# First-batch attention of a fused attention and MoE kernel: second q/k buffers, pooling on TensorE, and another order of the turns

## What is computed

```python
q_d = q.reshape(B, H, Sd, 4, D).mean(axis=3)     # k_d, v_d likewise
out_up = np.repeat(sm_attn(q_d, k_d, v_d), 4, axis=2)
mask = np.abs(pos[:, None] - pos[None, :]) < 4
attn = softmax(where(mask, scale * q @ k.T, -1e9))
x = (out_up + attn @ v).transpose(0, 2, 1, 3).reshape(1152, 512)
h = x @ w_in;  g = where(h > 0, h, exp(min(h, 0)) - 1);  x = g @ w_out
out = sum_e p[:, e] * (relu(x @ w1[e]) @ w2[e])
```

## Time and profile before

| | us |
|---|---|
| runs | 667.95, 667.06, 668.51; median 667.95 |
| profiled execution | 667.47, of which 665.4 are the span |
| start of the first pooled scores of pairs 0, 1 | 9.01, 16.96 |
| start of mix for pairs 0, 1, 2, 3 | 23.27, 32.20, 40.98, 47.49 |
| first layer-1 product, turn_in(4) | 49.18, 54.04 |

### The profile page before, as it was taken

The page is one execution under the profiler, slowest core; times in us unless marked ns, Lnnn a source line. Parts: engine busy times, 40 slices in busy tenths (PEclk is TensorE's granted clock), DMA queues, the critical chain, the costliest instruction groups (busy, mean ns, idle before and its releaser), DMA issues.

```text
span 665.4 us, 12923 instructions
## 1 busy us (share of the span) xinstructions
PE 651.9 (98%) x4750; PEld 599.6 (90%) x4756; DVE 324.4 (49%) x714; ACT 277.7 (42%) x759; POOL 304.5 (46%) x266
## 2 busy tenths in 40 slices
PE   7989999999999999999999999999999999999998
PEld 4768999999999999999989998998899899899886
DVE  4785454545444433465525435544454454365342
ACT  3766565656565653745214214233142162142110
POOL 3584343535359733878716326326138056061110
PEclk9999999999999999999999999999999999999999
DMA  9945070705112132111101103003003011010012
GB/s 181 242 74 163 4 199 4 196 1 162 66 53 76 65 104 84 64 64 65 64 1 64 65 0 123 3 0 126 0 13 113 0 63 63 1 64 0 1 48 95
DMA packets 51489, 46.11 MB, mean 69 GB/s; under 512 B 31616, under 2 KB 33920, under 8 KB 51456
## 3 DMA queue, kind: packets, MB, share of 16 engines
q1 hardware_dynamic: 51456, 45.67, 23.2%
HBM read 43.30 MB, written 2.36 MB: 69 GB/s over the span
## 4 chain that ended last, share of the span: by engine, by line
PE 88%; ACT 5%; DVE 5%; issue 1%; POOL 0%; ACTq 0%; DVEq 0%
PE psum L437 19%; PE psum L439 18%; PE psum L438 18%; PE psum L516 9%; PE psum L518 9%; PE psum L514 9%; ACT attn L670 2%; ACT attn_p L670 1%; DVE neg_max L901 1%; PE psum L355 1%; PE psum L342 1%; PE psum L429 1%; PE psum L408 1%; PE psum L374 1%; DVE sums L911 1%
## 5 line engine op out<-in xcount | busy, mean ns | idle before, releaser
L1162 POOL TENSOR_TENSOR wb_lo<-wb_raw,wb_hi 128x512 fp32r<-128x512 f32 x64 | 82.2, 1298 | 202.4 <-ACT wb_hi L702 202.4
L1028 DVE SCALAR_TENSOR_TENSOR o_acc<-psum,gate_now,o_acc 128x512 f32<-128x512 f32 x72 | 54.1, 751 | 125.6 <-PE psum L439 125.3
L439 PE MATMUL psum<-wb_hi,h_lo 128*128 128x512 f32 x288 | 112.3, 390 | 0.0
L438 PE MATMUL psum<-wb_lo,h_hi 128*128 128x512 f32 x288 | 112.2, 390 | 0.0
L437 PE MATMUL psum<-wb_hi,h_hi 128*128 128x512 f32 x288 | 112.0, 389 | 0.0
L759 ACT ACTIVATE h_hi<-psum 128x320 fp32r<-128x320 f32 (+1 forms) x128 | 52.4, 411 | 87.8 <-DVE psum L1000 40.4
L1162 POOL TENSOR_TENSOR wa_lo<-wa_raw,wa_hi 128x512 fp32r<-128x512 f32 x60 | 76.0, 1294 | 22.6 <-ACT wa_hi L746 14.1
L765 ACT COPY sums<-psum 128x256 f32<-128x256 f32 (+1 forms) x32 | 12.8, 400 | 156.4 <-PE psum L518 156.4
L437 PE MATMUL psum<-h_hi,wb_hi 128*128 128x288 f32 x256 | 76.8, 300 | 0.0
L439 PE MATMUL psum<-h_hi,wb_lo 128*128 128x288 f32 x256 | 75.4, 295 | 0.0
L438 PE MATMUL psum<-h_lo,wb_hi 128*128 128x288 f32 x256 | 75.4, 294 | 0.0
(11 more groups left out here) (146 smaller groups left out, 1539.4 us busy)
## 6 DMA issues: line engine op xcount, KB each, us to landing
wa_raw<-in_moe_w_in SPq DMA_DIRECT2D x8, 1024.0 KB, 5.7
wb_raw<-in_moe_w_out SPq DMA_DIRECT2D x8, 1024.0 KB, 5.1
wa_raw<-in_moe_w SPq DMA_DIRECT2D x8, 1024.0 KB, 4.9
wb_raw<-in_moe_w SPq DMA_DIRECT2D x8, 1024.0 KB, 5.0
out<-o_acc SPq DMA_DIRECT2D x9, 256.0 KB, 2.0
q_in<-in_q SPq DMA_DIRECT2D x10, 144.0 KB, 3.6
k_in<-in_k SPq DMA_DIRECT2D x10, 144.0 KB, 4.2
v_in<-in_v SPq DMA_DIRECT2D x5, 288.0 KB
```

The source lines that it names most:

```text
L438: nc.tensor.matmul(bank_cols, w_hi(n), x_lo_(n), start=False, stop=False)
L439: last = nc.tensor.matmul(bank_cols, w_lo(n), x_hi_(n), start=False, stop=(n == chunks - 1))
L1028: nc.vector.scalar_tensor_tensor(o_acc[:, m, :], psum[:, DOWN2_BANKS[(MT * half + m) % 2], :], gate_now[:, m:m + 1], o_acc[:, m, :], ALU.m ...
L1162: nc.gpsimd.tensor_tensor(lo[:, c, :], raw[:, c, :], hi[:, c, :].bitcast(F32), ALU.subtract).then_inc(lo_ready, 1)
```

## The change

Six things are done, all in mode ALONE. (1) qT, kT, qTs and kTs get a second copy, in y_acc, used by odd pairs. (2) The pooled q is made on TensorE: pool_in multiplies each q tile with pool4, a 96x24 matrix of ones in fours, into bank 2 from column 288; for pair 0 the pooled k too, into bank 3. VectorE makes pool4 from ident, and take_k reads the pooled q from PSUM; for pairs 1 to 3 it sums k as before. (3) The order: turn_in(u+2), turn_attn(u+1, 0) and score(u+2, 0) move a period ahead, and the orders of the other engines with them. (4) Outputs go to banks 4, 5 (pair 0), 6, 7 (pairs 1 and 2), 2, 3 (pair 3), and the last window's turn to bank 7 or bank 3, with other waits. (5) up_first is cut into open_groups: chunks 0 and 1 of two of the groups are issued ahead of pair 3's last span, the rest behind its mix. (6) The fillers ahead of the scores, around pair 3's turns and one near the start go. The core of it (slot(u) is u % 2 for the first batch, else 0; open_groups has the products of up_first for one chunk k and the groups named):

```diff
-LAST_BANK = {ALONE: 2, MIXED: 0}
+POOL_TOK = LT // FACTOR
+POOLED_BANKS = (2, 3)
...
-FILL_INPUTS, FILL_SUMS, FILL_ATTENTION, FILL_SCORES, FILL_TURNS, FILL_OUTPUTS = 9, 5, 6, 1, 1, 2
+FILL_INPUTS, FILL_SUMS, FILL_ATTENTION = 9, 5, 5
...
-    return ((4, 5) if u < HALF_PAIRS - 1 else (2, 3)) if mode == ALONE else (1, 3)
+    return ((4, 5), (6, 7), (6, 7), (2, 3))[u] if mode == ALONE else (1, 3)
+def last_at(u, mode):
+    if mode == MIXED:
+        return 0, 0
+    return (3, 128 * NPQ) if u == HALF_PAIRS - 1 else (7, HALF)
...
-        qT, kT = sb1("qT", [128, SEQ]), sb1("kT", [128, SEQ])
-        qTs, kTs = sb1("qTs", [128, PADDED]), sb1("kTs", [128, POOLED])
+        y_flat = y_acc[:].rearrange("p k n -> p (k n)")
+        qTs_at = 2 * SEQ
+        kTs_at = qTs_at + PADDED
+        qT, kT = (sb1("qT", [128, SEQ])[:], y_flat[:, 0:SEQ]), (sb1("kT", [128, SEQ])[:], y_flat[:, SEQ:qTs_at])
+        qTs = (sb1("qTs", [128, PADDED])[:], y_flat[:, qTs_at:kTs_at])
+        kTs = (sb1("kTs", [128, POOLED])[:], y_flat[:, kTs_at:kTs_at + POOLED])
...
+            def pool_in(n, src):
+                for c in range(NLT):
+                    at = POOLED_AT + POOL_TOK * c
+                    nc.tensor.matmul(psum[:, POOLED_BANKS[n], at:at + POOL_TOK], src[:, c, :], pool4[:], start=True, stop=True)
             def turn_in(u, mode):
                 if mode == MIXED:
                     pe.wait_ge(out_free, 2 * u + OUT_CREDIT)
                 for n, src in enumerate((q_in[held(u)], k_in[held(u)])):
                     pe.wait_ge((q_loaded, k_loaded)[n][held(u)], 32 * loads(u))
-                    if n == 1 and mode == ALONE and u >= 2:
-                        pe.wait_ge(attnT_p_copied, 2 * (u - 1))
-                        pe.wait_ge(attnT_copied, 3 * (u - 1) - 1)
+                    if mode == ALONE:
+                        if n == 0 and u >= 1:
+                            pe.wait_ge(qT_copied, u)
+                        if n == 1 and u == 1:
+                            pe.wait_ge(kT_copied, 1)
+                        if n == 1 and u >= 1:
+                            pe.wait_ge(pooled_ready, u)
+                        if n == 1 and u >= 2:
+                            pe.wait_ge(attnT_p_copied, 2 * (u - 1))
+                        if n == 1:
+                            pool_in(0, q_in[held(u)])
+                            if u == 0:
+                                pool_in(1, src)
...
-                if mode == ALONE and u > 0:
-                    fill(FILL_SCORES, bank)
+                if mode == ALONE and j == 1:
+                    pe.wait_ge(qT_copied, u + 1)
+                    pe.wait_ge(kT_copied, u + 1)
...
-                    pe.wait_ge(out_free, 2 * (u - 1) + j + OUT_CREDIT)
+                if mode == ALONE and u == 1:
+                    pe.wait_ge(out_free, j + OUT_CREDIT)
                 if j == 2:
-                    pe.wait_ge(attnT_p_copied, 2 * u + 1)
-                    nc.tensor.transpose(psum[0:WIN, LAST_BANK[mode], 0:128], attn[:, LAST, :], ident[:]
+                    if mode == MIXED:
+                        pe.wait_ge(attnT_p_copied, 2 * u + 1)
+                    elif u == HALF_PAIRS - 1:
+                        pe.wait_ge(attnT_p_copied, 2 * u + 2)
+                    else:
+                        pe.wait_ge(qT_copied, min(u + 3, HALF_PAIRS))
+                        if u == 2:
+                            pe.wait_ge(out_free, 2 * u + OUT_CREDIT)
+                    bank, at = last_at(u, mode)
...
+                    pe.wait_ge(qT_copied, HALF_PAIRS)
+                if mode == ALONE and u == 2:
+                    pe.wait_ge(out_free, 2 * u + OUT_CREDIT)
...
+            def open_groups(w, b, k, groups):
+                pe.wait_ge(wa_lo_ready, KC * w + k + 1)
+                pe.wait_ge(x_lo_ready, KC * b + k + 1)
+                for g in groups:
+                    if k == 0:
+                        bank_free1(w, g)
+                    cols, t = slice(128 * g, 128 * (g + 1)), slice(b * SEQ, b * SEQ + N1)
+                    bank = psum[:, MOE_BANKS[g], 0:N1]
+                    nc.tensor.matmul(bank, wa_hi[:, k, cols], x_hi[:, k, t], start=(k == 0), stop=False)
+                    nc.tensor.matmul(bank, wa_hi[:, k, cols], x_lo[:, k, t], start=False, stop=False)
+                    last = nc.tensor.matmul(bank, wa_lo[:, k, cols], x_hi[:, k, t], start=False, stop=(k == KC - 1))
+                    if k == KC - 1:
+                        last.then_inc(group_done, 1)
...
-            pe.wait_ge(ident_ready, 1)
+            pe.wait_ge(pool4_ready, 1)
             turn_in(0, ALONE)
             fill(FILL_SUMS, 5)
-            for j in range(3):
-                if j == 1:
-                    pe.wait_ge(band_ready, 1)
-                score(0, j, ALONE)
+            score(0, 0, ALONE)
+            pe.wait_ge(band_ready, 1)
+            score(0, 1, ALONE)
             turn_in(1, ALONE)
+            score(0, 2, ALONE)
             fill(FILL_ATTENTION, 5)
+            turn_attn(0, 0, ALONE)
+            score(1, 0, ALONE)
             for u in range(HALF_PAIRS):
-                for j in range(3):
-                    turn_attn(u, j, ALONE)
-                    if u + 1 < HALF_PAIRS:
-                        score(u + 1, j, ALONE)
-                    else:
-                        fill(FILL_TURNS, score_bank(HALF_PAIRS, 0, ALONE))
-                if u + 2 >= HALF_PAIRS:
-                    pe.wait_ge(exp_done, 3 * HALF_PAIRS - 1)
-                    fill(FILL_OUTPUTS, score_bank(HALF_PAIRS, 0, ALONE))
                 if u + 2 < HALF_PAIRS:
                     turn_in(u + 2, ALONE)
+                turn_attn(u, 1, ALONE)
+                if u + 1 < HALF_PAIRS:
+                    score(u + 1, 1, ALONE)
+                else:
+                    pe.wait_ge(out_free, 2 * u + OUT_CREDIT)
+                    open_groups(0, 0, 0, (2, 3))
+                    open_groups(0, 0, 1, (2, 3))
+                turn_attn(u, 2, ALONE)
+                if u + 1 < HALF_PAIRS:
+                    score(u + 1, 2, ALONE)
+                    turn_attn(u + 1, 0, ALONE)
+                if u + 2 < HALF_PAIRS:
+                    score(u + 2, 0, ALONE)
                 mix(u, ALONE)
+            open_groups(0, 0, 0, (0, 1))
+            open_groups(0, 0, 1, (0, 1))
+            open_groups(0, 0, 2, range(OPEN[0]))
+            turn_in(HALF_PAIRS, MIXED)
+            open_groups(0, 0, 3, range(OPEN[0]))
...
             copy_qT(0, ALONE)
-            for j in range(3):
-                exponentiate(0, j, ALONE)
+            exponentiate(0, 0, ALONE)
+            exponentiate(0, 1, ALONE)
             copy_qT(1, ALONE)
+            exponentiate(0, 2, ALONE)
+            exponentiate(1, 0, ALONE)
             for u in range(HALF_PAIRS):
-                for j in range(3):
-                    if j > 0:
-                        copy_attnT(u, j, ALONE)
-                    if u + 1 < HALF_PAIRS:
-                        exponentiate(u + 1, j, ALONE)
+                if u > 0:
+                    copy_pooled(u - 1, ALONE)
                 if u + 2 < HALF_PAIRS:
                     copy_qT(u + 2, ALONE)
-                copy_pooled(u, ALONE)
-                if u == 0:
+                if u > 0:
+                    split_x(u - 1, 0, u - 1)
+                copy_attnT(u, 1, ALONE)
+                if u == 1:
                     first_wa(0)
+                    first_wa(1)
+                if u == 2:
+                    first_wa(2)
                 if u + 1 < HALF_PAIRS:
-                    first_wa(u + 1)
-                split_x(u, 0, u)
+                    exponentiate(u + 1, 1, ALONE)
+                copy_attnT(u, 2, ALONE)
+                if u + 1 < HALF_PAIRS:
+                    exponentiate(u + 1, 2, ALONE)
+                if u + 2 < HALF_PAIRS:
+                    exponentiate(u + 2, 0, ALONE)
+            first_wa(3)
+            copy_pooled(HALF_PAIRS - 1, ALONE)
+            split_x(HALF_PAIRS - 1, 0, HALF_PAIRS - 1)
...
+                    def pooled(n):
+                        return psum[:, POOLED_BANKS[n], POOLED_AT:POOLED_AT + POOLED]
+                    def take_qTs():
+                        return nc.vector.tensor_scalar(qTs[slot(u)][:, 0:POOLED], pooled(0), HD ** -0.5, None, ALU.mult)
+                    def take_kT():
+                        nc.vector.tensor_copy(kT[slot(u)].rearrange("p (a n) -> p a n", a=2), k_turned).then_inc(kT_copied, 1)
+                    if u == 0:
+                        nc.vector.tensor_copy(kTs[slot(u)], pooled(1))
+                        take_qTs().then_inc(pooled_ready, 1)
+                        take_kT()
+                    else:
+                        take_qTs()
+                        take_kT()
+                        dve.wait_ge(kT_copied, u + 1)
+                        nc.vector.tensor_reduce(kTs[slot(u)], kT[slot(u)].rearrange("p (j r) -> p j r", r=FACTOR), X, ALU.add
```

(60 more changed lines are left out.)

36 lines of the change are left out of this document (10 added, 26 removed).

## The result

The changed kernel takes 674.88 us (four runs, 672.85 to 677.59) against 667.57 (four runs) for the kernel before: the ratio is 1.011, interval 1.007 to 1.0151. It is slower, by 7.3 us, outside the forecast range. The times of its four runs go with the mean clock that TensorE was granted in them: 0.997 in the run of 672.85, 0.995 in 673.89, 0.990 in 675.87, 0.987 in 677.59. The profiled execution is the first of these, 5.4 us above the profiled 667.47 of before; 4.5 of that lie in the span (669.9 against 665.4).

What follows compares the result with a forecast made beforehand. TensorE, busy 98% of the span, was taken as the bound, so only idle or filler time could be won. Profiled 667.47 less 0.95 gave 666.5, and 0.48 up to the runs' median gave 667.0; range 664.4 to 669.2.

Steps and rivals of the forecast that it cites:

- six pooling products per pair ... I take 0.5: TensorE's pooling of q in each pair: six products priced at 0.5 us together, between 0.2 and 0.8.
- The order and the loop: First-layer pairs: mix, copy, pooling, k turns, take, scores, mix again, about 9.5 us; mixes at 24.7, 34.3, 41.2, 48.2.
- The give-back behind the shared banks: Banks 2 and 3: pair 2's k turns wait for VectorE's copy; the 2 us lead is gone for window spans.
- ScalarE's series in the tail: Gap before the mix at 41.2: ScalarE's splits, copies and exponentials in series, behind outputs added only at 37.5.
- The 0.9 of gain: End of the attention part: front at 48.3 us instead of 49.18, counting 1.6 us of products done early.
- The tail: VectorE beside GpSimd's wa_lo subtractions: no long port hold, pair 2's outputs added at 45.1, last mix from 48.2.
- the two holds: VectorE in the tail, held on the port shared with GpSimd: charged 0.6 and 1.05 us.
- Rival 2: Tail, reciprocals of pair 3's last span: VectorE held 3.5 us by the shared ports, giving 669.5 us; chance 0.14.
- The five fillers: Opening, TensorE ahead of the first scores: fillers end at about 8.6 us, so scores start there instead of 9.0.
- Rival 3: TensorE's clock falls without the fillers; half a period at 1.2 GHz would give 671 us; chance 0.08.
- the stop at 16.5: TensorE idle from 16.45 to 18.0 us, waiting for VectorE's copy before pair 2's k turns.
- Rival 1: TensorE's pace decides: pooling at 0.2, periods of 8.2 us, 3.0 us won, giving 665.0 us; chance 0.31.

Runs made afterwards that it cites:

- the run with the late groups: Changed kernel with pooling back on VectorE and all four up groups opened behind pair 3's mix: 669.76 us, ratio 1.0029.

## Why the prediction was wrong

**The step that failed** is the term "six pooling products per pair ... I take 0.5", between ends of 0.2 and 0.8. It measured 1.36, above the upper end. The rows held the larger part of the answer: the earlier trace rows count 16 loads for a score pass whose code issues eight products (four windows, two heads). Plain f32 products show two passes a call in these traces, each with its own load of the weights; transposes show one (six calls, six rows). I took times per row and multiplied them by calls of the code. With the count doubled, the nearest row (0.09 us each) gives 1.1. The remaining 0.3 is that a pass took 0.113 to 0.118 us and not 0.09; why is open.

From there the working can be followed. Against the forecast the profiled run is later by 2.9 us at the first pooled scores (11.5 for 8.6) and by 3.8 at pair 1's (18.7 for 14.9); at the mixes by 4.3, 5.1, 5.4 and 5.5, and at the turn-in by 5.5 (58.63 for 53.1). As an estimate, 1.7 us of the 2.9 are pair 0's passes (twice 1.36 less 1.0) and about 1.2 are low clock and fillers. The three later poolings are 0.86 longer each than forecast, 2.6 together, which is what the lateness grows by from the first pooled scores to the turn-in, though not in equal steps. They sum to 5.5.

**The order and the loop** were right. With VectorE pooling the mixes start at 24.78, 34.35, 41.90 and 48.68 against my 24.7, 34.3, 41.2 and 48.2, and the turn-in at 53.64 against 53.1. Some of this nearness is luck: that run has neither the 0.5 of pooling nor the take of 1.8, but a take of three rows of 0.75 to 0.76, and the two differences nearly cancel. The terms of the loop also sum to 8.9 to 9.3, not to the 9.0 to 9.4 that I wrote; that changes nothing here. The give-back behind the shared banks, the new loop through the waiting copy and ScalarE's series in the tail are all there; cutting the loop's wait and then the copy in the tail gained what was forecast in kind. The 0.9 of gain was 0.4 in that profile.

**The tail** was right in kind: no VectorE row of 3 us came; the two holds cost 0.6 and 0.7 beyond the 0.16 that the row takes alone (rows of 0.78 and 0.85). Rival 2 didn't happen.

**"The five fillers" cost nothing** was priced as cover under VectorE's sums. With those sums gone, the fillers were on the path, for about 1.3 us at the low clock (from 10.2 to 11.5). Yet taking them out was worse.

**Rival 3, the clock, came true**, with 0.08 of chance and in another place: not at the stop at 16.5, but already behind the first pooling passes, and in other runs again near 24 and 36 us. By the times it is 2 of the 7.3 us (the median of 674.88 less the lowest run of 672.85), besides some 1.2 within the profiled run. The low level is not the changed kernel's alone: three of sixteen runs of the kernel before had 0.997 and took 1 to 2 us longer than the rest. By the Trainium skill, page TensorE: Matmul & The Clock Gate, section "Part 4: PE-mode transpose", transposes don't count as busy the way products do. No loss by that shows in the run with VectorE pooling: it has the same turns and fewer fillers than before, its profile held its level, and no run was above 668.21. The low stretch from 19.4 us in the run with the late groups, which has the same turns up to there, leaves the matter open. Rival 1 rested on pooling at 0.2, which measured 1.36.

What stays open is why the clock falls in some runs and not in others of one kernel, such as the kernel with pair 0 on VectorE.

## What to carry to other kernels

Before pricing a new product from a row, divide the count in the row by the calls in the code: f32 products that aren't transposes count double here, and 24 columns didn't make them cheap: the twelve weight loads of a pooling fill 1.41 us, as long as the passes themselves. When work is added to an engine that is 94% busy in that stage, expect most of its time on the path (7.05 us of 7.6 with fillers), less what the engine that gives it up no longer does. Test the part that moves work apart from the part that reorders it. Give a change that thins out TensorE's work several timed runs with their clocks, since one profile shows one draw. And where a clock column reads 1.00 near the start, check it against the duration of an instruction that you know at both levels.

## What was not expected of the hardware

The granted clock can fall to its lower level while TensorE is busy without a gap: behind 24 passes of 24 columns, the rows show 1.00 busy per microsecond and a clock of 0.50. With fillers of 512 columns in the same places, the mean clock was 0.999 or 1.0 in all four runs. In the changed kernel the mean clock goes with the time, from 0.997 and 672.85 us to 0.987 and 677.59; in the run with VectorE pooling, clocks of 0.996 to 1.0 lie within 666.60 to 668.21 in no order. And in one profile TensorE stayed at the low level from its start until about 17 us, in a stretch that the trace's clock record doesn't cover, so that neither the clock column nor the mean of 0.995 shows it.
